# A new order for all five queues of a chunk-select attention with a gated MLP

## The chip, the cores and the metric

The kernel runs on one core of one Trainium2 chip. The metric is the device time in microseconds (us) of one execution.

## The reference

Four batches of 768 positions and 512 features. First an attention of 8 heads of 64, then an MLP block on its output:

```python
k_min, k_max = k_chunks.min(3), k_chunks.max(3)          # 24 chunks of 32 keys
ub = sum(maximum(q * k_min, q * k_max))                  # upper bound of q.k in a chunk
top_chunks = argsort(where(causal, ub, -1e9))[..., -6:]  # 6 chunks for each query
attn = softmax(where(sel & causal, q @ k.T / 8, -1e9)) @ v
x = attn with its heads side by side                     # (4, 768, 512)
u, v = split(gelu(x @ w_in))                             # 512 and 512
v_s = w_sg @ (layernorm(v) * g_ln) + b_sg                # over the 768 positions
out = x + (u * v_s) @ w_out                              # float32
```

## The kernel before

The program is written out by hand as 1267 operations. `_build` makes them in the order in which they are thought, each with its engine, a tag and what it reads and writes; `TABLE` then gives, for each of the five queues (PE, ACT, DVE, POOL, SP), the list of operation numbers in the order in which that engine runs them, the PSUM bank of each of PE's output tiles (`slots`), and the engine of those operations that can run on more than one (`engine`). `place` takes the lists as they are, `link` works out which waits on semaphores the order needs, and `emit` writes each queue. An engine runs its queue strictly in order: an instruction that waits holds up all that stand behind it on that engine.

The work goes by 16 pairs of heads (four pairs to a batch) and, behind each fourth pair, by batch. The tags that this text uses:

- Loads on SP's queue: `kn`, `qn`, `vn` (a pair's keys, queries, values, three buffers each). A buffer comes free when its last reader is done: that of `vn_11` with `vcast_8`.
- `kmm`, `kred` (L596, L613, DVE): minimum and maximum of each chunk of 32 keys; `wsub` (L601, DVE) makes the difference that the bounds product uses. `ktr`, `qtr` (PE) and `kev`, `qev` (ACT or DVE, L375 and L378): keys and queries turned and copied out of PSUM. `rel` (L375 on ACT, L377 on POOL and DVE): max(q, 0).
- `ub` (L696, PE): the upper bounds. `m8` (L713, L763), `dn` (L719, L768), `dt` (L723, L771), all DVE: the eight largest, the comparison of the bounds with the sixth, and the turning of its result; `qd` copies that result into the operand `QA` of the scores.
- `kcast`, `qcast`, `kcp`, `vcast`: casts to bf16 and copies, most of them on POOL (L378). `kT` (L623): the keys turned by a transposing transfer on SP's queue.
- `sc` (L812, PE) the scores, `exp` (L818, L873, ACT), `aff` (L823, POOL) the causal part of the mask on the diagonal blocks, `pv`, `pvd` (L896, L903, PE) the product with the values, `rcp` and `xs` (L911, L919) the division.
- `dt_x` (L927): the attention output turned by a transposing transfer on SP's queue, four for each of batches 1 and 2 and two for batch 3 (`dt_x_1_0` to `dt_x_1_3`).
- `hv`, `hu` (L950, L990, PE): the two halves of x @ w_in, with gelu on ACT (L954, L995). The layer norm of v is a chain on two engines: `bns`, `bna` (L959, L961, DVE) the statistics of six tiles, `var` (L963, DVE), `rstd` (L965, POOL, the power -0.5), `nmr` (L967, DVE), then six `vhat`, the normalised tiles, on ACT (L973) or DVE (L978).
- `pt` (L1007, PE): w_sg times `vhat`; each of its groups reads all six tiles. `vs`, `gt` (L1013, L1017, DVE): bias and gate. `ou` (L1030, PE), `os` (L1036, DVE), `st` (L1043, SP or ACT): w_out, the residual, the store.

A tag ends with the pair or batch and the part: `vhat_1_3` is tile 3 of batch 1, `qd_10_1` the second head of pair 10. The products of one batch are interleaved with the scores of the next batch's pairs, so all engines work on two or three pairs and a batch at once.

Of the kernel before, what the change touches and what calls it, by code (L numbers as in the profile page):

```python
# [258 lines left out]
def _build(nc, ctx, q, k, v, w_in, g_ln, w_sg, b_sg, w_out, out):  # L259
# [852 lines left out]
    for p in range(4, NP + 4):  # L1112
# [21 lines left out]

TABLE = {
# [15 lines left out]
    "act": (  # L1151
# [10 lines left out]
    "dve": (  # L1162
# [16 lines left out]
    "pool": (  # L1179
# [12 lines left out]
    "slots": (  # L1192
        "7314540635701767417545434327664501450123017623544450145016745767215354160145450101237305501452301450141"
        "3253136406153734136267206061520463145674567016732310123452345454774213567016723450104250167014523675763"
        "4121051765072355610147332155450467672345454554370167016723234216644167010123230123066767010167451752414"
        "3511004157267361266727074160101676723234301234523674575454523452367750012301014501435654023273353454272"
        "4540161502447"),
    "engine": (
# [10 lines left out]
}  # L1209


# [56 lines left out]
```

How the kernel before makes its waits and increments, by code:

```python
        def run(e, eng):  # L186
            for i in self.order[e]:
                o = ops[i]
                need = {}
                for d in o.waits:
                    p = ops[d]
                    s = dsem[p.dma] if p.dma is not None else sems[p.eng]
                    key = p.dma if p.dma is not None else p.eng
                    if key not in need or need[key][1] < p.count:
                        need[key] = (s, p.count)
                for s, c in need.values():
                    eng.wait_ge(s, c)
                ins = o.fn(eng)
                if o.dma is not None:
                    ins.then_inc(dsem[o.dma], 16)
                elif o.inc:
                    ins.then_inc(sems[e], 1)
            if e == "sp":
                for d, idxs in self.dma_sems.items():
                    if ops[idxs[-1]].tag[0] == "st":
                        eng.wait_ge(dsem[d], 16 * len(idxs))
```

## Time and profile before

| | us |
|---|---|
| median of 3 runs | 216.65 (216.13 to 218.79) |
| the profiled execution | 217.55 |
| its span, as the profile measures it | 215.4 |
| mean granted clock of TensorE | 0.992 of full speed |
| busy in that span: PE, DVE, ACT, POOL | 194.8, 185.5, 163.7, 132.8 |

The profile is that of one execution. Its rows give the start in the span and the duration in us; "xN" is the number of instructions that a row groups. A bracket at the end of a row holds the time for which the engine sat idle before it and, behind the arrow, the instruction that ended the wait. In a window's row the busy time of each engine stands ahead of its number of instructions; the granted clock is a share of full speed; a DMA share of 1 is all 16 DMA engines busy. SPq and ACTq are the queues that issue transfers; their rows last as long as the issue takes, not the transfer.

### The profile page before, as it was taken

To read this page: it belongs to the slowest core of one execution; us is meant where nothing else is said; L and a number is where in the kernel's file an instruction comes from. 1 tells how busy PE (TensorE), PEld (TensorE's weight loads), DVE (VectorE), ACT (ScalarE), POOL (GpSimd) and SP (SyncE) were. 2 spreads that over 40 slices of the span, in tenths; PEclk is the share of its full clock that TensorE was granted. 3 is DMA by queue.
4 is the path that set the end of the run, shared out by engine and by line. 5 is a ranking of instruction groups with operands and counts; after the bars stand their busy time and mean duration, and the time that the engine had idled before them with its cause. 6 is when DMAs were issued, how large, how long until landed. Compare 5 with 4: busy or idle time off the path is not lost.

```text
span 215.4 us, 6383 instructions
## 1 busy us (share of the span) xinstructions
PE 194.8 (90%) x2549; PEld 126.0 (58%) x2564; DVE 185.5 (86%) x531; ACT 163.7 (76%) x247; POOL 132.8 (62%) x168
## 2 busy tenths in 40 slices
PE   7778897899999999997959989998995999999993
PEld 2445676745766577763535757873572677655652
DVE  3899999798999999969889999987779664888994
ACT  3559998799999999977795889979685698765010
POOL 5447699798799999994596795987059016002000
PEclk9999999999999999999999999999999799999999
DMA  7999999999998999999895838698500213103117
GB/s 147 218 221 252 213 214 336 227 270 257 198 235 189 229 203 215 200 171 195 177 219 117 190 76 203 130 173 203 104 3 2 53 35 88 49 0 127 70 49 243
DMA packets 96801, 35.02 MB, mean 163 GB/s; under 512 B 91514, under 2 KB 92292, under 8 KB 96772
## 3 DMA queue, kind: packets, MB, share of 16 engines
q1 hardware_dynamic: 95908, 33.70, 73.5%
q10 hardware_dynamic: 864, 0.92, 1.3%
q8 instruction: 20, 0.33, 0.7%
q14 instruction: 9, 0.07, 0.1%
HBM read 24.38 MB, written 6.29 MB: 142 GB/s over the span
## 4 chain that ended last, share of the span: by engine, by line
PE 44%; DVE 35%; ACT 11%; issue 3%; DMA 3%; POOL 2%; SPq 0%; DVEq 0%
PE PS L1007 8%; PE PS L950 8%; PE PS L812 7%; PE PS L1030 7%; DVE PS L1013 3%; DVE vhat L978 3%; PE PS L896 3%; DVE Bn L613 3%; DVE uT L1017 3%; PE PS L990 3%; DVE XS L919 3%; ACT vgb L954 2%; ACT E L873 2%; PE PS L696 2%; DVE KA L378 2%
## 5 line engine op out<-in xcount | busy, mean ns | idle before, releaser
L818 ACT ACTIVATE E<-PS 128x1024 bf16<-128x1024 f32 (+1 forms) x72 | 62.3, 924 | 9.2 <-PE PS L812 8.5
L1007 PE MATMUL PS<-wsgT,vhat 128*128 128x384 bf16 x192 | 35.9, 334 | 5.1 <-DVE vhat L978 4.7
L812 PE MATMUL PS<-QA,KA 128*128 128x128 bf16 (+2 forms) x336 | 36.1, 247 | 0.4 <-DVE rden L911 0.3
L812 PEld LDWEIGHTS PS<-QA,KA 128*128 128x128 bf16 x336 | 23.9, 98 | 10.9 <-ACT E L818 1.8
L823 POOL TENSOR_SCALAR_AFFINE_SELECT E<-E 128x768 bf16<-128x768 bf16 x24 | 20.4, 864 | 13.5 <-ACT E L818 12.8
L1007 PEld LDWEIGHTS PS<-wsgT,vhat 128*128 128x128 bf16 x192 | 18.3, 100 | 17.3 <-issue 6.2
L378 POOL CAST QA<-qT 64x768 bf16<-64x768 f32 (+1 forms) x27 | 22.2, 826 | 7.1 <-DVE qT L378 3.8
L995 ACT ACTIVATE uT<-PS 128x384 bf16<-128x384 f32 x32 | 15.1, 505 | 12.8 <-PE PS L990 12.7
L990 PE MATMUL PS<-xT,winb 128*128 128x384 bf16 x128 | 23.1, 326 | 0.0
L950 PE MATMUL PS<-winb,xT 128*128 128x512 bf16 x92 | 20.8, 379 | 2.4 <-issue 0.9
L873 ACT ACTIVATE E<-PS 128x1024 bf16<-128x1024 f32 (+1 forms) x24 | 20.5, 926 | 2.6 <-PE PS L858 2.4
L1030 PE MATMUL PS<-woutb,uT 128*128 128x512 bf16 (+1 forms) x98 | 21.8, 353 | 0.6 <-issue 0.2
L1013 DVE SCALAR_TENSOR_TENSOR PS<-PS,bgT,bsgbc 128x384 f32<-128x384 f32 x32 | 19.2, 614 | 2.3 <-PE PS L1007 2.3
L965 POOL TENSOR_TENSOR rstd<-rstd,neghalf 128x6 f32<-128x6 f32 x4 | 5.4, 1348 | 24.8 <-DVE rstd L963 24.8
L896 PE MATMUL PS<-vx,E 128*128 128x65 bf16 x480 | 19.3, 194 | 0.4 <-issue 0.4
L959 DVE BATCH_NORM_STATS2 stats<-vgb 128x6 f32<-128x512 f32 x24 | 16.0, 683 | 3.9 <-ACT vgb L954 3.8
L613 DVE TRANSPOSE_TENSOR_REDUCE Bn<-kn 128x24 f32<-128x768 f32 x20 | 18.9, 957 | 0.0
L1036 DVE TENSOR_TENSOR osb<-PS,XS 128x512 f32<-128x512 f32 x21 | 14.2, 681 | 4.9 <-PE PS L1030 3.2
L896 PEld LDWEIGHTS PS<-vx,E 128*128 128x128 bf16 x480 | 16.9, 98 | 2.0 <-issue 0.8
L1017 DVE TENSOR_TENSOR uT<-PS,uT 128x384 bf16<-128x384 f32 x32 | 17.4, 550 | 0.6 <-ACT uT L995 0.2
L990 PEld LDWEIGHTS PS<-xT,winb 128*128 128x128 bf16 x128 | 12.1, 98 | 8.6 <-ACT vgb L954 0.2
L919 DVE TENSOR_TENSOR XS<-PS,rden 128x384 bf16<-128x384 f32 x30 | 16.3, 550 | 0.5
(121 smaller groups left out, 388.3 us busy)
## 6 DMA issues: line engine op xcount, KB each, us to landing
qn<-in_q_dram SPq DMA_DIRECT2D x32, 192.0 KB, 5.2
vn<-in_v_dram SPq DMA_DIRECT2D x16, 384.0 KB, 5.3
out_dram<-osb SPq DMA_DIRECT2D x20, 256.0 KB, 2.6
kn<-in_k_dram SPq DMA_DIRECT2D x10, 384.0 KB, 5.9
kn<-in_k_dram SPq DMA_DIRECT2D x12, 192.0 KB, 4.5
uT<-in_moe_w_sg_dram SPq DMA_DIRECT2D x4, 384.0 KB, 5.9
vgb<-in_moe_w_in_dram SPq DMA_DIRECT2D x3, 512.0 KB, 7.7
vhat<-in_moe_w_sg_dram SPq DMA_DIRECT2D x2, 384.0 KB, 3.8
```

Of the source, the lines that this page charges most:

```text
L378: return e.tensor_copy(dst(), src())
L613: P.op("dve", lambda d, m=m, op=op: d.tensor_reduce(Bn[u][:, x, m, :], kn[s][:].rearrange("p i t d -> p (i t d)").rearrange("p (c x) -> p ...
L812: r = e.matmul(both(ts)[:, o:o + n], KA[w][i][:, 128 * kb:128 * kb + 128], QA[w][i][:, q0:q0 + n], start=True, stop=True)
L818: P.op("act", lambda e, ts=ts, c0=c0, c1=c1, i=i: e.activation(E[es][:, i, c0:c1], both(ts)[:, 0:c1 - c0], ACTF.Exp, scale=SCALE), act(c1 ...
L873: P.op("act", lambda e, ts=ts, c0=c0, c1=c1, n=n: e.activation(E[es][:, :, c0:c1], both(ts).rearrange("p (i x) -> p i x", i=2)[:, :, 0:n], ...
L896: r = e.matmul(t.ap()[:, 65 * qb:65 * qb + 65], E[es][:, i, a:a + 128], vx[w][:, kb, i, :], start=first, stop=False, skip_group_check=True)
L950: r = e.matmul(t.ap()[:, 0:F], xT[s][:, dk, 128 * qt:128 * qt + 128], winb[:, dk, F:DFF], start=(dk == 0), stop=(dk == NDK - 1))
L990: r = e.matmul(t.ap()[:, 0:TG], winb[:, dk, 128 * fb:128 * fb + 128], xT[s][:, dk, TG * tg:TG * tg + TG], start=(dk == 0), stop=(dk == NDK ...
L1007: r = e.matmul(t.ap()[:, 0:TG], vhat[s][:, sb, 128 * fb:128 * fb + 128], wsgT[:, sb, TG * tg:TG * tg + TG], start=(sb == 0), stop=(sb == N ...
L1013: P.op("dve", lambda d, t=t, fb=fb, tg=tg: d.scalar_tensor_tensor(t.ap()[:, 0:TG], t.ap()[:, 0:TG], bgT[:, NT + fb:NT + fb + 1], bsgbc[:, ...
L1017: P.op("dve", lambda d, t=t, fb=fb, tg=tg: d.tensor_tensor(gT[s][:, fb, TG * tg:TG * tg + TG], t.ap()[:, 0:TG], uT[s][:, fb, TG * tg:TG * ...
L1030: r = e.matmul(t.ap()[:, 0:c1 - c0], gT[s][:, fb, 128 * qt:128 * qt + 128], woutb[:, fb, c0:c1], start=(fb == 0), stop=(fb == NF - 1))
```

## The change

Only `TABLE` changes. The operations themselves are the same 1267, with the same operands and tiles. The lists of all five queues stand in a new order, PSUM banks are given anew to the tiles, and the engine of 74 operations changes: 18 from POOL to ACT, 15 from ACT to DVE, 14 from ACT to POOL, 14 from DVE to ACT, 6 from DVE to POOL, 4 from POOL to DVE, and three stores of the last batch from ACT's queue to SP's. The queues hold 338, 235, 403, 164 and 127 operations before (PE, ACT, DVE, POOL, SP), 338, 235, 402, 162 and 130 after. At the same place in their queue stand 85 of PE's, 24 of ACT's, 53 of DVE's, 16 of POOL's, 23 of SP's; the others move by 1, 3, 2, 3 and 2 places in the median and by at most 15, 17, 50, 31 and 20.

The lists are rows of numbers; the lines of DVE and POOL around the layer norms of batches 1 and 2 (735 is `var_1`, 736 `rstd_1`, 737 `nmr_1`, 738 to 743 `vhat_1_0` to `vhat_1_5`, 1007 `rstd_2`):

```diff
-        "593 595 510 688 699 698 700 687 695 713 717 714 718 721 696 725 722 726 729 733 730 734 735 697 737 743 742 "
-        "740 741 701 686 761 702 762 782 767 783 788 768 764 765 705 789 791 792 770 875 822 823 826 771 692 690 693 "
...
+        "510 685 688 699 698 695 700 717 829 713 714 721 718 725 722 726 729 696 733 730 734 735 697 701 737 741 740 "
+        "742 739 686 702 782 783 687 761 788 767 762 764 789 768 765 791 792 875 770 822 771 823 692 677 690 693 876 "
...
-        "418 657 353 635 539 396 619 626 664 578 606 681 584 607 540 824 674 637 643 579 736 644 815 547 683 870 638 "
-        "704 833 832 863 682 586 645 684 808 703 913 853 827 872 906 677 846 948 922 865 871 834 893 866 957 941 964 "
-        "930 965 894 1086 1109 873 1007 1079 977 978 931 980 932 1102 966 960 1125 1149 1156 1132 967 1192 "),
...
+        "545 353 396 626 619 664 657 608 606 578 683 674 643 607 584 637 824 540 547 638 863 644 736 704 684 605 703 "
...
+        "929 965 1086 1079 1109 924 925 873 980 966 977 1007 1125 1102 1132 979 1156 1149 967 1192 "),
```

The same with tags, for the places that the prediction comes to ("..." for what lies between):

```
DVE, pairs 0, 1    before  ... utr_0_0 m8_0_0 init_13 dn_0 wsub_1_1 wsub_1_0 dt_0 ...
                   after   ... wsub_1_0 utr_0_0 wsub_1_1 m8_0_0 dn_0 qev_2_0 dt_0 ...
rel_0, rel_1       before  on ACT        after  on POOL
first loads of SP  the same 34 in both orders, qn_0 issued 2nd and 4th, before 4th and 5th
SP, batch 1        before  dt_x_1_0 st_0_1 dt_x_1_1 dt_x_1_2 dt_x_1_3 kT_10 vn_8
                   after   kT_10 kn_13 qn_12_1 dt_x_1_0 dt_x_1_1 dt_x_1_2 dt_x_1_3 vn_8
                           (st_0_1 earlier)
SP, vn_11          before  vn_8 qn_13_0 qn_13_1 qn_14_0 kn_14 qn_14_1 vn_10 st_0_5 vn_9 kn_15 kT_11 vn_11
                   after   vn_8 qn_13_0 kT_11 qn_15_0 qn_14_1 qn_13_1 kn_14 qn_14_0 vn_11
POOL, batch 1      before  kcast_12 kcast_11 kcp_10_1 qcast_10_0 kcp_9_0 rstd_1 qcast_10_1 aff_8_1 vcast_8
                           qcast_11_1 rel_13 kcp_10_0 qd_10_1 ... vcast_11
                   after   kcast_12 kcp_8_0 vcast_8 kcp_10_0 kcast_13 qcast_10_1 rstd_1 qd_10_1 vcast_11 qd_8_0
DVE, batch 1       before  var_1 m8_10_0 nmr_1 vhat_1_5 vhat_1_4 vhat_1_2 vhat_1_3 dn_10 kred_12_1 ... dt_10
                   after   var_1 m8_10_0 dn_10 nmr_1 vhat_1_3 vhat_1_2 vhat_1_4 vhat_1_1 kred_12_1 ... dt_10
PE, batch 1        before  pt_1_0_0 pt_1_1_0 pt_1_0_2 sc_9_1_1 sc_8_0_1 pt_1_1_2 pt_1_0_1 sc_8_0_2
                   after   sc_9_1_1 pt_1_1_0 pt_1_0_0 pt_1_1_2 pt_1_0_2 sc_8_0_2
SP, batch 2        before  dt_x_2_2 dt_x_2_3
                   after   dt_x_2_2 kT_15 st_1_1 kT_14 dt_x_2_3
POOL, batch 2      before  rstd_2 aff_12_0 qd_14_0 qd_14_1 qcast_14_1 qd_15_1 vcast_14 aff_13_0 qcast_15_1
                   after   vcast_13 qd_15_1 qcast_15_1 qd_14_0 rstd_2 aff_14_0 aff_13_0 aff_14_1
DVE, batch 2       before  bna_2_4 bna_2_5 var_2 dt_14 nmr_2 and four vhat_2 (3, 1, 5, 4)
                   after   dt_14 ... bna_2_5 bna_2_4 var_2 nmr_2 and four vhat_2 (0, 5, 3, 2)
PE, batch 2        after   all six hv_2 ahead of the first hu_2
```

## Rows read from the trace of the kernel before

**Rows 1.** The page's first part: busy us (share of the span) and instructions of each engine.

```profile
PE 194.8 (90%) x2549; PEld 126.0 (58%) x2564; DVE 185.5 (86%) x531; ACT 163.7 (76%) x247; POOL 132.8 (62%) x168
```

**Rows 2.** Windows: stretch, length, engines' busy us (count), granted clock, DMA share, GB/s.

```profile
0.00:44.00 44.00, 36.55 (x678) 24.06 (x681) 37.59 (x125) 32.49 (x45) 30.74 (x50) 1.00 1.09 226
62.50:99.00 36.50, 34.78 (x607) 24.05 (x608) 34.43 (x108) 33.29 (x46) 32.98 (x40) 1.00 1.10 201
99.00:112.60 13.60, 10.95 (x67) 5.77 (x68) 11.94 (x41) 11.28 (x22) 9.20 (x11) 1.00 0.97 207
162.00:164.00 2.00, 0.00 (x0) 0.00 (x0) 2.00 (x3) 1.97 (x4) 1.83 (x3) 1.00 0.00 0
165.95:169.36 3.41, 3.41 (x18) 1.95 (x17) 2.29 (x6) 1.01 (x6) 1.43 (x2) 0.50 0.00 0
```

**Rows 3.** Chain of waits, around both gaps of the middle: start, us, engine, work.

```profile
96.29 2.83 DMA xT<-XS
...
108.70 3.87 DVE vhat L978 x4
...
160.51 3.52 DVE vhat L978 x4
```

**Rows 4.** Timeline of PE; in brackets the idle time before and who ended it.

```profile
13.83 0.69 PE L696 MATMUL PS<-qT,Wall 64*32 64x288 f32 x8 [1.26 <-DVE Wall L601]
...
99.39 1.46 PE L950 MATMUL PS<-winb,xT 128*128 128x512 bf16 x6 [0.89 <-DMA xT<-XS]
...
112.71 3.08 PE L1007 MATMUL PS<-wsgT,vhat 128*128 128x384 bf16 x18 [2.37 <-DVE vhat L978]
...
164.17 1.14 PE L1007 MATMUL PS<-wsgT,vhat 128*128 128x384 bf16 x6 [2.32 <-DVE vhat L978]
...
165.78 1.98 PE L1007 MATMUL PS<-wsgT,vhat 128*128 128x384 bf16 x6 [0.29 <-DVE XS L919]
```

**Rows 5.** Groups by line and shape: busy us, mean ns | idle time before.

```profile
L377 POOL TENSOR_SCALAR rT<-qT 128x576 f32<-128x576 f32 x8 | 13.9, 1735 | 0.9 <-DVE Wall L649 0.4 <-POOL QA L378 0.3
...
L375 ACT ACTIVATE rT<-qT 128x576 f32<-128x576 f32 x7 | 4.8, 713 | 0.8 <-DVE qT L378 0.7
```

**Rows 6.** Timeline of SP's queue, batch 1: start, us to issue, line, transfer.

```profile
93.22 4.35 SPq L927 DMA_TRANSPOSE xT<-XS  x3
97.61 1.29 SPq L623 DMA_TRANSPOSE KA<-kbx  x1
...
116.87 0.57 SPq L539 DMA_DIRECT2D vn<-in_v_dram  x1
```

**Rows 7.** Timeline of DVE around the three normalisations and one compare.

```profile
56.05 0.72 DVE L768 TENSOR_TENSOR Dn<-U,m 128x576 bf16<-128x576 f32 x1
...
159.66 0.81 DVE L967 SCALAR_TENSOR_TENSOR nmr<-mv,rstd 128x6 f32<-128x6 f32 x1 [0.79 <-POOL rstd L965]
160.51 3.52 DVE L978 TENSOR_SCALAR vhat<-vgb,mv,rstd 128x512 bf16<-128x512 f32 x4
...
195.50 1.92 DVE L978 TENSOR_SCALAR vhat<-vgb,mv,rstd 128x512 bf16<-128x512 f32 x4
```

**Rows 8.** Timeline of POOL around rstd of batches 0, 1 and 2.

```profile
55.34 1.35 POOL L965 TENSOR_TENSOR rstd<-rstd,neghalf 128x6 f32<-128x6 f32 x1 [1.84 <-DVE rstd L963]
...
107.10 1.36 POOL L965 TENSOR_TENSOR rstd<-rstd,neghalf 128x6 f32<-128x6 f32 x1 [2.28 <-DVE rstd L963]
108.52 0.83 POOL L378 CAST QA<-qT 64x768 bf16<-64x768 f32 x1
...
111.38 0.90 POOL L378 CAST QA<-qT 64x768 bf16<-64x768 f32 x1
...
158.28 1.35 POOL L965 TENSOR_TENSOR rstd<-rstd,neghalf 128x6 f32<-128x6 f32 x1 [8.63 <-DVE rstd L963]
...
160.52 1.46 POOL L378 COPY QA<-Dt 32x576 bf16<-32x576 bf16 x2
```

**Rows 9.** The page's DMA issues, loads of v: count, KB each, us to landing.

```profile
vn<-in_v_dram SPq DMA_DIRECT2D x16, 384.0 KB, 5.3
```

More of the change, by code:

```diff
@@ L1136 @@
     "pe": (
[14 rows of a table removed]
-    "act": (
[9 rows of a table removed]
[14 rows of a table added]
+    "act": (
[9 rows of a table added]
         "1266 1251 "),
     "dve": (
[16 rows of a table removed]
-    "pool": (
[12 rows of a table removed]
-    "slots": (
[L1193 to L1197, printed above, removed]
-    "engine": (
[10 rows of a table removed]
[16 rows of a table added]
+    "pool": (
[12 rows of a table added]
+    "slots": (
+        "7254656104434567504750772235464501012301677623016016701016745325470430630145450101017052723452367450110"
+        "0632431631273611473015324140741676101452367016757500123236701455667542367010123450107236701452345456213"
+        "0167411761064565137546367356757401230101014567322323012301454227105445010123230123546767670167453253544"
+        "0732021663474654776725266760101456723675701014501014563010123234545723014523234501504140357004712753102"
+        "4132546056116"),
+    "engine": (
[10 rows of a table added]
 }
```

111 rows, old and new, of the table TABLE are left out of this document.

## The prediction

> **What bounds the kernel now.** I read the busy shares first [rows 1]: TensorE (PE) is busy for 194.8 of 215.4 us, so a new order of the same work can only win back what PE loses in some 20 us of gaps, or keep the other engines from being the ones that make them. The profiled execution took 217.55 us: 215.4 us of span and 2.15 us around it. The sum below is made against 217.55; the median of the three runs, 216.65, lies 0.90 below it, and I carry that 0.90 over at the end.
>
> The stretches come next [rows 2]. Here the reader is to see that the gaps have places. In the first 44 us PE is busy for 36.55, at a DMA share of 1.09, so this stretch is fed by transfers that are already back to back. From 62.5 to 99 us PE, DVE, ACT and POOL are all busy for over 32.9 of 36.5 us: here every order meets a full engine. The rest comes down to two places in the middle: 99 to 112.6, where PE misses 2.65 us, and 162 to 164, where PE does nothing at all while DVE (2.00), ACT (1.97) and POOL (1.83) are all full. Behind the second gap stands a stretch of 3.41 us in which PE works without a pause at a granted clock of 0.50.
>
> The chain of waits [rows 3] says who holds the end at these places: a transposing transfer (xT) of batch 1, and twice the four DVE instructions `vhat` (the normalisation of v, line 978), 3.87 and 3.52 us. PE's own timeline [rows 4] prices the waits: 1.26 us at 13.83 for `Wall`, 0.89 at 99.39 for xT, 2.37 at 112.71 and 2.32 at 164.17 for `vhat`, and 0.29 at 165.78.
>
> **The change, part by part.** Instructions and bytes are the same but for 74 that run on another engine; by their groups' mean durations that is +0.8 us for ACT, -0.3 for DVE and -3.2 for POOL, against the busy times of [rows 1] nothing that bounds. So each term is a wait that appears or goes. The last digit of a name is the part of it (`vhat_1_3`: batch 1, tile 3; `kT_10`: head pair 10).
>
> 1. *Head.* The wait of 1.26 us [rows 4] is for `wsub_1`, which stands on DVE behind a top-8, a mask operation and a compare of pair 0; the new order puts it ahead of them: at best -1.25. Against it, `rel_0` and `rel_1` go from ACT to POOL, 1735 ns instead of 713 [rows 5], so the bounds product that needs them is ready up to 1.0 later (+1.0). The first 34 loads are the same set in both orders and the DMA share is full, so the end of the stretch can't come much earlier whatever PE does. I take half of the gain, **-0.6, between -1.25 and +1.0**.
>
> 2. *xT of batch 1.* hv of batch 1 waits for the last of four `dt_x_1` on SP's queue, which issues them from 93.22 with no gap [rows 6]; `kT_10`, 1.29 us, stood behind them and now stands ahead of all four. hv is late by that unless SP finds a gap before: **+1.0, between 0 and +1.29**.
>
> 3. *`vhat` of batch 1.* Four of them took 3.87 us from 108.70 and 3.52 from 160.51 [rows 3], but 1.92 from 195.50 [rows 7]. What differs is POOL [rows 8]: four casts and selects lie beside the first (108.52, the last at 111.38), two copies and more beside the second (160.52), nothing beside the third. In the new order the instruction behind `rstd_1` on POOL is `qd_10_1`. It needs `dt_10`, which stands on DVE behind the four `vhat`; so POOL must stand idle while they run. They end 3.87 - 1.92 = 1.95 earlier, and PE's first product that reads them has a score group (`sc_9_1_1`, moved ahead) to fill what is left of the 2.37: **-2.0, between -2.4 (the whole wait and no more) and 0**. Where the cover goes: the casts that stood beside `vhat` now stand ahead of `rstd_1`, which is term 4.
>  The compare `dn_10` also moves, from behind the `vhat` to between `m8_10_0` and `nmr_1`, so it runs beside `rstd_1`. Cost 0: `dn` of an earlier pair ran at 56.05 beside `rstd_0` (55.34 to 56.69) in 0.72 us, with `rstd_0` no longer than the others (1.35; 1.36 at 107.10) [rows 7, 8]. The Trainium skill, "SBUF — State Buffer", section "Who interferes with whom", says that a DVE instruction with two inputs in SBUF and a GpSimd instruction that reads SBUF lock each other out for a whole instruction; by that rule `dn_10` and `rstd_1` would run one after the other, and the sum would be -4.4. These two rows overlap by 0.64 us, so by them the trace doesn't agree for this pair, though by term 3's rows it does for `vhat`.
>
> 4. *`rstd_1` on POOL* now has four casts and copies ahead of it that stood behind or elsewhere (`vcast_8`, `kcp_10_0`, `kcast_13`, `qcast_10_1`), 0.83 us each by the row at 108.52, 3.3 in all. POOL sat idle for 2.28 us ahead of `rstd_1` [rows 8], which leaves 1.0; some of the four can run earlier still: **+0.4, between 0 and +0.9**.
>
> 5. *hv of batch 2.* On SP `kT_15` and `kT_14` (1.29 each by the one at 97.61 [rows 6]) now lie ahead of the last `dt_x_2`. The first can hide in a queue that is slack there; the two can't both: **+0.4, between 0 and +1.3**.
>
> 6. *`vhat` of batch 2.* Behind `rstd_2` POOL now has three causal selects that wait for exponentials, which ACT can give only after the gelus of this batch and a change of its table; the two selects, two copies and two casts that stood there go ahead of `rstd_2`, into 8.63 us in which POOL waited [rows 8], or behind. So POOL is idle beside these four as well: 3.52 - 1.92 = 1.6, and `nmr_2`, 0.81 for six numbers in a row [rows 7], lay beside a select and falls by some 0.6. `dt_14` leaves the place ahead of `nmr_2`, and all hv now come before all hu, so the statistics end earlier. Together that exceeds the wait of 2.32 and the one of 0.29 at 165.78 [rows 4], so both go whole: **-2.6, between -2.6 and 0**.
>
> 7. *Clock.* The 3.41 us at 0.50 [rows 2] come right behind the 2 us in which PE did nothing. Without the gap they would take half: **-1.7, between -1.7 and 0**.
>
> 8. *Elsewhere.* Between the named places the instructions move by one to three places in the median, in stretches that are full: 0. The most to win in 62.5 to 99 is DVE's 2.07 us of idle time [rows 2]; the most to lose at one new wait is what the largest old one in such a stretch costs, 1.26 [rows 4]. The tail is 0: three stores go from ACT's queue to SP's, the last chain (product, add, store) is the same.
>
> Sum: -0.6 + 1.0 - 2.0 + 0.4 + 0.4 - 2.6 - 1.7 = **-5.1**, so 217.55 - 5.1 = 212.45 for an execution like the profiled one, and **211.5** for the median.
>
> **The rivals.**
>
> *POOL in order, waiting for a load.* `vcast_11` now stands ahead of `qd_8_0`, which the score group `sc_8_0_2` needs and PE reaches near 115.6 (110.7 for the first product of batch 1, then five groups at some 1 us, as the 18 matmuls from 112.71 are three in 3.08 [rows 4]). The load of vn_11 was issued at 116.87 [rows 6] and such loads land 5.3 us later [rows 9]: 122.2, and with the cast (0.83) and the copy (half of the 1.46 at 160.52) 123.8: PE stands for 8.2 us. 211.5 + 8.2 = 219.7, and if the clock falls to 0.50 behind such a gap as it did at 165.95, 1.7 more: **219.7 to 221.4**, slower than before. For it: POOL is in order, and vn_11 sits in a buffer that is free only after `vcast_8`, which is itself late on POOL. Against it: on SP the load stands ahead of a store and three loads that preceded it before. It decides if vn_11 lands after about 114.
>
> *The transfers take it back.* Terms 1, 2, 4 and 5 all at their upper ends: +1.0, +1.29, +0.9, +1.3 in place of -0.6, +1.0, +0.4, +0.4, which is +3.3: **214.8**. For it: SP issues without a gap before 99.4, and the loads run at a share over 1 up to then [rows 2]. Against it: four upper ends at once.
>
> *The gaps are refilled.* What PE wins at 112 and 164 it waits for at the next product, since DVE was busy for 11.94 of 13.60 us ahead of the first and full in the second [rows 2], and its work is the same: **216.6**, no change. Against it: DVE's own time falls here, as the `vhat` get shorter by 3.5 us.
>
> *`dn_10` and `rstd_1` one after the other.* If they shut each other out as `vhat` and the casts seem to, `nmr_1` is late by the 0.72 us of a compare, and so are the `vhat`: **212.2**. For it: the `vhat` rows; against it: the overlap of 0.64 us at 56.05. The page's rule of term 3 is this case.
>
> **How the numbers follow.** A median more than 2% off, which is about what a measurement of this kernel can tell from no change, is below 212.3 or above 221.0. The forecast has 0.47 and a range of its own from 208.0 to 213.5: the low end is terms 1, 3, 6 and 7 at their lower and 2, 4 and 5 at zero, -7.95, so 208.7, and 0.7 for the spread of the runs (the fastest of the three lies 0.52 below the median). Of the 0.47, 0.43 lies below 212.3. The compare beside `rstd_1` has 0.11, half of it (0.06) below 212.3; the transfers have 0.19, the refilled gaps 0.11, the load behind POOL 0.12, half of it above 221.0. Faster 0.43 + 0.06 = 0.49; same 0.04 + 0.05 + 0.19 + 0.11 + 0.06 = 0.45; slower 0.06. The range leaves out the slow rival (0.12) and little else: 208.0 to 216.8.
>
> **What would show it.** Terms 3 and 6: the four `vhat` rows near 1.9 us with no POOL row beside them, and PE's waits for `vhat` under 0.5. Term 7: no stretch of 0.50 near 166. Term 1: no wait for `Wall` near 13.8. Terms 2 and 5: a wait of PE for xT at the first hv of batches 1 and 2, longer than 0.89 in batch 1. Term 4: `rstd_1` starting more than 0.2 us after its variance. The slow rival: a wait of several us near 115 for a POOL copy to QA. It would be wrong if the `vhat` stay long with POOL idle, or if the time won at 112 is lost again before 149.

## The result and the profile after

The changed kernel took **209.28 us** (median of 4 runs, 207.63 to 211.59) beside 216.43 for the kernel before: a ratio of 0.9621, interval 0.9521 to 0.9722. The forecast was 211.5 in a range of 208.0 to 216.8. Two more sets of four runs of the same kernel gave 210.48 (0.9764, 0.9723 to 0.9804) and 210.92 (0.9745, 0.9686 to 0.9804), so all twelve have a median of 210.5: about 6 us under before, where the sum was 5.1. The ratios are those of the fast runs alone and so not the quotients of the medians, and the profile of a_cover1, told below, is of a slow run (219.30 us against that kernel's median of 214.70), so only its waits are read. The profiled execution below is the fastest of the twelve, 207.63 us with a span of 205.6; where it flatters the change, the later profiles say so.

Page of the changed kernel, first part, as [rows 1]:

```profile
PE 191.6 (93%) x2564; PEld 124.8 (61%) x2564; DVE 177.7 (86%) x530; ACT 163.3 (79%) x245; POOL 129.2 (63%) x166
```

Windows, columns as [rows 2]; the first two lie where rows 2 have a gap of PE, the third covers the head:

```profile
99.00:112.60 13.60, 13.52 (x88) 7.43 (x86) 12.03 (x35) 11.94 (x22) 6.29 (x8) 1.00 1.10 226
149.30:166.00 16.70, 16.70 (x174) 11.44 (x173) 13.87 (x34) 14.70 (x23) 5.43 (x8) 1.00 0.01 2
0.00:44.00 44.00, 36.31 (x684) 24.53 (x685) 36.32 (x125) 35.24 (x50) 33.69 (x52) 1.00 1.08 229
```

PE misses 0.08 us in the stretch where it missed 2.65, and nothing from 149.3 to 166, at full clock: both gaps of the middle are gone, and so is the stretch at 0.50 (1.2 of TensorE's 2.4 GHz). The wait for xT, which lay in part inside the first window, now lies ahead of it (below). The head is as it was (36.31 against 36.55 us busy).

Chain of waits, as [rows 3]:

```profile
95.10 2.82 DMA xT<-XS
98.01 3.63 PE PS L950 x16
105.72 1.36 POOL rstd L965
```

The `vhat` have left the chain's long pieces; the transfer of xT is still there.

Timeline of PE, as [rows 4]:

```profile
13.91 0.69 PE L696 MATMUL PS<-qT,Wall 64*32 64x288 f32 x8 [0.18 <-POOL rT L377]
...
98.01 1.24 PE L950 MATMUL PS<-winb,xT 128*128 128x512 bf16 x5 [2.28 <-DMA xT<-XS]
...
109.59 4.06 PE L1007 MATMUL PS<-wsgT,vhat 128*128 128x384 bf16 x24
...
156.70 3.57 PE L1007 MATMUL PS<-wsgT,vhat 128*128 128x384 bf16 x21
```

The first products of batches 1 and 2 (109.59, 156.70) wait for nothing. The wait of 1.26 us for `Wall` is now one of 0.18 for POOL's `rel_1`, at the same time of day (13.91 against 13.83). The wait for xT has grown from 0.89 to 2.28.

Timelines of DVE and POOL, as [rows 7, 8]:

```profile
106.31 0.76 DVE L768 TENSOR_TENSOR Dn<-U,m 128x576 bf16<-128x576 f32 x1
107.11 0.17 DVE L967 SCALAR_TENSOR_TENSOR nmr<-mv,rstd 128x6 f32<-128x6 f32 x1
107.32 1.92 DVE L978 TENSOR_SCALAR vhat<-vgb,mv,rstd 128x512 bf16<-128x512 f32 x4
...
154.63 1.92 DVE L978 TENSOR_SCALAR vhat<-vgb,mv,rstd 128x512 bf16<-128x512 f32 x4
...
185.89 1.92 DVE L978 TENSOR_SCALAR vhat<-vgb,mv,rstd 128x512 bf16<-128x512 f32 x4
```

```profile
105.72 1.36 POOL L965 TENSOR_TENSOR rstd<-rstd,neghalf 128x6 f32<-128x6 f32 x1 [1.74 <-DVE rstd L963]
110.84 0.65 POOL L378 COPY QA<-Dt 32x576 bf16<-32x576 bf16 x1 [3.76 <-DVE Dt L771]
111.56 0.82 POOL L378 CAST vx<-vn 128x768 bf16<-128x768 f32 x1
...
153.05 1.35 POOL L965 TENSOR_TENSOR rstd<-rstd,neghalf 128x6 f32<-128x6 f32 x1 [2.89 <-DVE rstd L963]
```

All three sets of four `vhat` take 1.92 us. POOL is idle beside the first two: 3.76 us ahead of `qd_10_1` (110.84), nothing behind `rstd_2` at 153.05 until 162. `dn_10` (106.31) ran inside `rstd_1` (105.72 to 107.08) in 0.76 us, and `nmr_1` followed 0.03 us behind `rstd_1`.

SP's queue, as [rows 6]: `kT_10`, then, behind a load of keys and one of queries (`kn_13`, `qn_12_1`), the four `dt_x_1`.

```profile
85.70 1.22 SPq L623 DMA_TRANSPOSE KA<-kbx  x1
...
90.05 6.34 SPq L927 DMA_TRANSPOSE xT<-XS  x4
```

To see which stages moved, I count along PE's queue, which has 338 operations in either order: the table gives the time between the ends of its operations 159, 174, 189, 204, 264 and 279, from the traces of the kernel before, of three executions of the changed one and of three experiments told below (b_head differs from before by two moves on DVE). At each of these places the two orders have run the same operations but for at most one. The stages are the head, batch 0 and the attention of batch 1; hv of batch 1; its hu and its first products; its next products among scores; up to the end of hu of batch 2; the first products of batch 2; the rest.

| | to 159 | 174 | 189 | 204 | 264 | 279 | 338 |
|---|---|---|---|---|---|---|---|
| before | 93.3 | 12.3 | 13.5 | 8.7 | 33.3 | 13.5 | 37.6 |
| b_head | 96.6 | 11.1 | 13.5 | 8.7 | 33.2 | 11.9 | 37.6 |
| changed | 91.5 | 13.0 | 10.6 | 7.6 | 33.3 | 9.0 | 37.5 |
| a_again | 94.9 | 12.8 | 10.7 | 7.6 | 33.5 | 9.0 | 37.5 |
| a_again2 | 94.8 | 12.8 | 10.6 | 7.6 | 33.5 | 8.9 | 37.5 |
| b_pool2 | 93.9 | 11.1 | 14.9 | 8.6 | 33.5 | 9.3 | 37.6 |
| b_three | 93.8 | 11.0 | 11.2 | 8.6 | 33.8 | 9.3 | 37.6 |

From the third column on, executions of one kernel agree within 0.2 us, but for stretches at half the clock (before at 279; b_pool2 at 189). The changed order wins 2.8 at 189, 1.1 at 204, and 3.0 at 279 (against 11.9; the 13.5 holds the stretch at 0.50 as well). It loses 0.5 to 2.0 at 174, behind xT. The first column varies by 3 us between executions of one kernel (91.5 to 94.9), more than the orders differ.

### The profile page after: what moved, and what is told of

Same layout as the page of the kernel before. It is cut to its first block, busy times and chain, and to the rows that moved or that the text cites. A ratio compares the mean times of both kernels' runs of the same rounds, so it can differ in the third digit from the quotient of the medians.

```text
span 205.6 us, 6389 instructions
## 1 busy us (share of the span) xinstructions
PE 191.6 (93%) x2564; PEld 124.8 (61%) x2564; DVE 177.7 (86%) x530; ACT 163.3 (79%) x245; POOL 129.2 (63%) x166
## 4 chain that ended last, share of the span: by engine, by line
PE 56%; POOL 14%; DVE 13%; ACT 7%; issue 4%; DMA 3%; SPq 1%; POOLq 0%; DVEq 0%
PE PS L950 10%; PE PS L1007 9%; PE PS L812 8%; PE PS L990 7%; PE PS L1030 5%; POOL QA L378 5%; PE PS L896 5%; ACT E L873 4%; POOL E L823 3%; PE PS L743 2%; PE PS L567 2%; DMA qn<-in_q_dram 2%; DVE uT L1017 2%; PE PS L903 2%; DVE PS L1013 2%
## 5 line engine op out<-in xcount | busy, mean ns | idle before, releaser
L1007 PE MATMUL PS<-wsgT,vhat 128*128 128x384 bf16 x192 | 34.2, 326 | 0.0
L950 PE MATMUL PS<-winb,xT 128*128 128x512 bf16 x96 | 21.7, 379 | 3.0 <-DMA xT<-XS 2.3
L1030 PE MATMUL PS<-woutb,uT 128*128 128x512 bf16 (+1 forms) x108 | 24.0, 355 | 0.0
L995 ACT ACTIVATE uT<-PS 128x384 bf16<-128x384 f32 x32 | 14.0, 489 | 10.4 <-PE PS L990 10.3
L378 POOL CAST QA<-qT 64x768 bf16<-64x768 f32 (+1 forms) x24 | 20.2, 842 | 3.0 <-DVE qT L378 1.2
L378 POOL COPY QA<-Dt 32x576 bf16<-32x576 bf16 x23 | 15.2, 662 | 8.1 <-DVE Dt L771 6.3
L954 ACT ACTIVATE vgb<-PS 128x512 f32<-128x512 f32 x24 | 13.8, 594 | 6.5 <-PE PS L950 6.3
L950 PEld LDWEIGHTS PS<-winb,xT 128*128 128x128 bf16 x96 | 9.0, 98 | 14.2 <-issue 2.9
L919 DVE TENSOR_TENSOR XS<-PS,rden 128x384 bf16<-128x384 f32 x31 | 16.8, 546 | 0.5
```

Of the source, the lines that this page charges most:

```text
L378: return e.tensor_copy(dst(), src())
L950: r = e.matmul(t.ap()[:, 0:F], xT[s][:, dk, 128 * qt:128 * qt + 128], winb[:, dk, F:DFF], start=(dk == 0), stop=(dk == NDK - 1))
L1007: r = e.matmul(t.ap()[:, 0:TG], vhat[s][:, sb, 128 * fb:128 * fb + 128], wsgT[:, sb, TG * tg:TG * tg + TG], start=(sb == 0), stop=(sb == N ...
L1030: r = e.matmul(t.ap()[:, 0:c1 - c0], gT[s][:, fb, 128 * qt:128 * qt + 128], woutb[:, fb, c0:c1], start=(fb == 0), stop=(fb == NF - 1))
```

## Experiments

Numbers in the diffs are operations, as in the change. Labels with a_ start from the changed kernel, with b_ from the kernel before.

**1. The changed kernel again** (a_again, a_again2; no edit).

> The changed kernel once more, unchanged, beside the other runs. The profiled execution of it took 207.63 us at a granted clock of 0.999, two others 209.18 and 209.38 at 0.992. Theory: the 1.6 us between them is one stretch of some 3.4 us at half the clock, which comes in some executions and not in others; so a run here lies near 207.6 or near 209.3, and a profile at 0.992 shows one stretch at 0.50 behind a wait of PE. Rival: the runs at 209.3 wait for transfers somewhere, and their lower clock is spread over the span: then no single stretch at 0.50.

> The changed kernel unchanged, as the measure for the other three runs beside it. Expected 209 to 211 us, 2.3 to 3.5 per cent under the kernel before, and in the profile PE's wait for xT at the first hv of batch 1 between 1.5 and 2.8 us.

Measured: 210.48 and 210.92. Both profiles have a clock of 0.991 or 0.992. Windows of the first (columns as before), and its PE timeline:

```profile
8.00:10.00 2.00, 0.65 (x13) 0.48 (x12) 1.32 (x6) 0.84 (x2) 1.91 (x1) 1.00 1.35 218
...
12.00:14.00 2.00, 2.00 (x16) 0.55 (x8) 0.55 (x3) 1.54 (x3) 1.65 (x1) 0.50 1.35 218
```

```profile
101.21 5.12 PE L950 MATMUL PS<-winb,xT 128*128 128x512 bf16 x23 [2.08 <-DMA xT<-XS]
```

One stretch at 0.50, as the theory had it, but in the head, behind 8 to 10 us in which PE was busy for 0.65 of 2.00 us. The theory's price failed: all eight runs lie between 210.00 and 211.48, and two of them (210.26 and 210.00) had a clock of 1.0, so the clock alone does not part 207.63 from the others. Against the fastest execution a_again's PE is 1.0 us late at its 17th operation, behind that stretch, and 3.4 at its 159th; what made the other 2.4, at full clock, is open. And the wait for xT stands at 101.21, 3.2 us later than in the fastest execution, since PE came to it that much later.

**2. POOL's work put back beside `vhat` of batch 2** (a_cover2).

```diff
 pool
-924 925 873 980 966 977 1007 1125
+924 873 1007 925 980 966 977 1125
```

> The changed kernel with four of POOL's copies and casts (kcp_14_0, qd_15_1, qcast_15_1, qd_14_0, some 3 us) moved from ahead of rstd_2 to behind it, so that they lie beside the four vhat of batch 2 again; nothing else. My theory (a vhat on DVE and a cast or copy on POOL shut each other out): the four vhat go from 1.92 us to between 3.2 and 3.8, PE waits 1.3 to 1.9 us ahead of the first product of batch 2, the time is up by that, and by 1.7 more if the clock falls behind the wait. Rival (the gain of batch 2 came from the statistics, which end earlier because all hv stand ahead of hu): vhat stay under 2.3 or PE does not wait, and the time is up by less than 0.5 us.

Measured: 212.48, 2.0 above the a_again measured beside it. DVE, POOL and PE:

```profile
158.48 0.17 DVE L967 SCALAR_TENSOR_TENSOR nmr<-mv,rstd 128x6 f32<-128x6 f32 x1 [1.47 <-POOL rstd L965]
158.69 3.51 DVE L978 TENSOR_SCALAR vhat<-vgb,mv,rstd 128x512 bf16<-128x512 f32 x4
```

```profile
158.51 0.83 POOL L378 COPY KA<-INDF 64x768 bf16<-64x768 bf16 x1
...
161.17 0.74 POOL L378 COPY QA<-Dt 32x576 bf16<-32x576 bf16 x1
```

```profile
162.34 3.90 PE L1007 MATMUL PS<-wsgT,vhat 128*128 128x384 bf16 x23 [1.47 <-DVE vhat L978]
```

Four copies and casts on POOL, and the same `vhat` take 3.51 us; PE waits 1.47, both inside the theory's numbers. The time, up by 2.0, is 0.1 above the theory's 1.9, and the stage of the table's column 279 took 10.5 us against 9.0. So the earlier statistics alone don't carry the gain.

**3. The same for batch 1** (a_cover1, then a_cover1b).

```diff
 pool, a_cover1
-547 638 863 644 736 704
+547 736 638 863 644 704
 pool, a_cover1b
-824 540 547 638 863 644 736 704
+824 547 644 736 540 638 863 704
```

> The changed kernel with three of POOL's copies and casts (kcp_10_0, kcast_13, qcast_10_1, 2.5 us) moved from ahead of rstd_1 to behind it, beside the four vhat of batch 1; nothing else. My theory: the four vhat 3.0 to 3.6 us instead of 1.92, PE's first product of batch 1 waits for them some 1.0 to 1.5 us, time up by 1.0 to 1.5. Rival (the gain of batch 1 came from the score group that now stands ahead of the products, or from hv): vhat may get longer, but the time stays within 0.5 us.

Measured: 214.70, 4.2 above a_again, three times what I expected; the profile names the rest. ACT, then PE:

```profile
116.76 0.49 ACT L375 ACTIVATE qT<-PS 128x384 f32<-128x384 f32 x1 [3.79 <-POOL QA L378]
```

```profile
117.69 2.49 PE L990 MATMUL PS<-xT,winb 128*128 128x384 bf16 x8 [3.05 <-ACT uT L995]
```

The moved `qcast_10_1` frees the tile that ACT's next copy (`qev_13`) writes. ACT stood 3.79 us for it with the gelus behind, and PE 3.05 us for those. That the kernel's other runs have the same waits is inferred, from the next run, which has neither these waits nor a loss of that size. There I took this cast out:

> As a_cover1, but kcp_8_0 in place of qcast_10_1 goes behind rstd_1 (with kcp_10_0 and kcast_13), so that nothing moved frees a buffer that ACT or PE wait for. Theory (a_cover1 lost 1.0 to 1.5 us to the longer vhat and the rest to ACT, which waited 3.79 us for qcast_10_1): vhat of batch 1 about 3.3 us, PE waits 1 to 1.5 us, and the time is up by 1.0 to 1.6 against a_again's 210.48, not by 4.

Measured: 210.23 (209.11 to 211.75), no loss seen against 210.48 (another set of runs of before, 216.41 beside 216.32). DVE and PE:

```profile
107.70 3.32 DVE L978 TENSOR_SCALAR vhat<-vgb,mv,rstd 128x512 bf16<-128x512 f32 x4
```

```profile
111.17 4.06 PE L1007 MATMUL PS<-wsgT,vhat 128*128 128x384 bf16 x24 [0.88 <-DVE vhat L978]
```

The lock-out is there (3.32 us), the wait is 0.88 rather than 1.0 to 1.5, and a median of four runs that spread over 2.6 us can't show it. In the profile the stage of column 189 took 11.7 us against 10.6, so the loss is there, at the low end of the theory's 1.0 to 1.6. The `vhat` grew by 1.40 and the wait by 0.88; hu and a score group cover the difference.

**4. Casts added where there were none** (a_vhat3).

```diff
+    for n in range(4):
+        P.op("pool", lambda g: g.tensor_copy(kbx[0][:].rearrange("p i t -> p (i t)"), qT[0][:]), gps(S), ("junk", n),
+             reads=[("qT", 0, 0), ("qT", 0, 1)], writes=[("kbx", 0)])
 pool
-1192
+1192 1267 1268 1269 1270
```

> The changed kernel with four casts of 128x768 float32 to bf16 added on POOL right behind rstd_3, reading a tile that is done with and writing another, so that they lie beside the four vhat of batch 3, where POOL had nothing to do; their result is used by nothing. Theory: the four vhat go from 1.92 to 3.3 to 3.9 us, as those of batches 1 and 2 did beside other casts, and PE's first product of batch 3 is late by 1.4 to 1.9; nothing behind it can give that back: time up by that. Rival (the vhat of batches 1 and 2 were long for another reason, such as the transfers or the scores beside them): 1.92 to 2.3 us, time up by under 0.4.

Measured: 212.02, 1.5 above a_again. DVE, POOL, PE, and the window behind:

```profile
186.51 0.77 DVE L967 SCALAR_TENSOR_TENSOR nmr<-mv,rstd 128x6 f32<-128x6 f32 x1 [0.85 <-POOL rstd L965]
187.32 3.49 DVE L978 TENSOR_SCALAR vhat<-vgb,mv,rstd 128x512 bf16<-128x512 f32 x4
```

```profile
186.44 3.63 POOL L1133 CAST kbx<-qT 128x768 bf16<-128x768 f32 x4
```

```profile
190.95 8.66 PE L1007 MATMUL PS<-wsgT,vhat 128*128 128x384 bf16 x42 [2.07 <-DVE vhat L978]
```

```profile
190.00:195.00 5.00, 4.05 (x16) 2.03 (x17) 3.06 (x6) 0.00 (x0) 0.07 (x1) 0.70 0.01 3
```

From 1.92 to 3.49 us with nothing else changed. Even `nmr_3`, six numbers to a row, took 0.77 beside the first cast and takes 0.17 without. PE's wait of 2.07, where the changed kernel has none, is a little over the theory's 1.4 to 1.9, and was followed by a stretch at a lower clock, as in [rows 2].

**5. One part alone on the kernel before** (b_pool2).

```diff
 pool
-873 1007 1079 977 978 931 980 932 1102 966 960
+873 1079 977 978 931 980 966 932 1007 1102 960
 dve: 976 (dt_14) from ahead of 1008 to behind 975
```

> The kernel before with one part of the change alone: on POOL aff_12_0, qd_14_0, qd_14_1, qcast_14_1, qd_15_1, qcast_15_1 and vcast_14 moved ahead of rstd_2, and on DVE dt_14 moved to behind dn_14, since the copies read it. My theory: the four vhat of batch 2 fall from 3.52 to about 1.9 us, nmr_2 from 0.81 to 0.2, PE's wait of 2.32 us at the first product of batch 2 falls under 0.5, the stretch at half the clock goes: 2 to 4 us faster than before. Rival (the order of hv and hu is needed too): PE still waits over 1.5 us, and the time is within 1 us of before.

Measured: 213.39, ratio 0.9881 (0.9830 to 0.9931), 2.9 under before. DVE and PE:

```profile
160.54 0.17 DVE L967 SCALAR_TENSOR_TENSOR nmr<-mv,rstd 128x6 f32<-128x6 f32 x1 [1.47 <-POOL rstd L965]
160.75 1.92 DVE L978 TENSOR_SCALAR vhat<-vgb,mv,rstd 128x512 bf16<-128x512 f32 x4
```

```profile
112.09 4.24 PE L1007 MATMUL PS<-wsgT,vhat 128*128 128x384 bf16 x16 [2.37 <-DVE vhat L978]
...
162.81 1.14 PE L1007 MATMUL PS<-wsgT,vhat 128*128 128x384 bf16 x6
```

Eight operations moved, and batch 2's gain is there: 162.81 waits for nothing. The row at 112.09 is the untouched batch 1: same wait of 2.37, and this time the clock fell behind it (16 matmuls in 4.24 us; 18 took 3.08 in [rows 4]).

**6. Three parts together** (b_three).

```diff
 pool, besides b_pool2
-579 736 644 815 547 683 870 638 704 833
+579 644 547 736 704 815 683 870 638 833
 dve, besides b_pool2
-697 737 743 742 740 741 701 686 761 702 762
+697 701 737 743 742 740 741 686 702 761 762
-823 826 771 692 690 693 691 876
+823 692 690 693 691 826 771 876
```

> The kernel before with three local moves only: the one of b_pool2 for batch 2 (213.39 beside 216.32); the like for batch 1 (POOL: qcast_10_1 and vcast_8 ahead of rstd_1, qd_10_1 right behind it; DVE: dn_10 ahead of nmr_1, dt_10 behind kred_12_1); and on DVE the four small steps of the bounds of pair 12 (wcp_12, wsub_12) ahead of kcp_12_1 and gt_1_0_3, as PE waited 0.82 us for them at 126.61. Theory (the gain of the change is these three waits, and nothing comes from the rest): vhat of batch 1 1.92 us, PE's waits at 112.7 and 126.6 under 0.5 each, time 5 to 6 us below before, that is within 1 us of the changed kernel. Rival (a large part comes from the order everywhere else): at most 4 us below before.

Measured: 211.55, ratio 0.9795 (0.9703 to 0.9887): 4.9 under before, between the two theories' numbers and nearer to the first; some 1 us above the changed kernel. The interval, 2.4 to 6.4 us, holds both theories; the table decides, with 2.3 won at 189 (13.5 to 11.2) and 2.6 at 279 (11.9 to 9.3). DVE and PE:

```profile
107.80 1.92 DVE L978 TENSOR_SCALAR vhat<-vgb,mv,rstd 128x512 bf16<-128x512 f32 x4
```

```profile
109.87 3.08 PE L1007 MATMUL PS<-wsgT,vhat 128*128 128x384 bf16 x18 [0.41 <-DVE vhat L978]
...
123.09 0.36 PE L903 MATMUL PS<-vx,E 128*128 128x65 bf16 x6 [0.67 <-POOL E L823]
...
126.79 0.61 PE L812 MATMUL PS<-QA,KA 128*128 128x384 bf16 x4 [0.80 <-DVE U L752]
```

The `vhat` of batch 1 take 1.92 us, and the wait for them fell to 0.41. The wait for the bounds of pair 12 went too, but 0.67 and 0.80 us of other waits (for a select on POOL, for DVE's transposes) took its place, so the table's column 204 stays at 8.6: that third move gained nothing.

**7. The head alone** (b_head).

```diff
 dve
-82 63 64 20 65 86 83 66
+82 83 63 86 64 20 65 66
```

> The kernel before with DVE's wsub_1_0 moved ahead of utr_0_0 and wsub_1_1 ahead of m8_0_0, as in the change; nothing else. Term 1 of the prediction gave this move 0.6 to 1.25 us. My reading of the dependences now: the bounds of pair 1 also need rel_1, which ends 13.56 where wsub_1 ends 13.78, so PE's wait of 1.26 us falls by 0.2 to 0.3 alone and the time stays within 0.5 of before. Rival (term 1): the wait falls under 0.3, the time by 0.6 or more.

Measured: 217.08, ratio 1.0019 (0.9984 to 1.0054). PE, the end of `wsub_1` on DVE, and `rel_1` on ACT:

```profile
13.71 0.69 PE L696 MATMUL PS<-qT,Wall 64*32 64x288 f32 x8 [1.12 <-DVE Dn L719]
```

```profile
11.86 0.13 DVE L601 TENSOR_TENSOR Wall<-PS,Wall 128x12 f32<-128x12 f32 x1
```

```profile
12.88 0.68 ACT L375 ACTIVATE rT<-qT 128x576 f32<-128x576 f32 x1
```

`wsub_1` ended at 11.99 instead of 13.78, and PE still waited 1.12 us. In the program this product waits on `wsub_1` and `rel_1` alone, and `rel_1` ended at 13.55 before and 13.56 here; the row names another DVE instruction that happened to end last before it.

**8. kT_10 behind the transposes, and two repairs** (a_kT10, a_best, a_warm).

```diff
 sp, a_kT10
-647 636 673 648 552 612 650 710 421
+647 673 648 552 612 650 710 636 421
 sp, a_best
-647 636 673 648 552 612 650 710 421 707 675 896 837 708 835
+647 673 648 552 612 650 710 707 708 636 421 675 896 837 835
 pe, a_best and a_warm
-4 80 89 62 5 117
+4 5 80 89 62 117
```

> The changed kernel with kT_10 on SP's queue moved back from ahead of the four dt_x_1 to behind them; nothing else. Theory (term 2: SP issues in order, so kT_10 makes xT late): dt_x_1_3 is issued some 1.2 us earlier, PE's wait at the first hv of batch 1 falls from 2.1 to 2.8 us to about 1.0 to 1.5, the time falls by 0.8 to 1.3 (more where the clock fell behind that wait). Rival (the last division, or ACT, holds xT back): the wait and the time stay within 0.4.

Measured: 210.13. PE:

```profile
98.75 2.53 PE L950 MATMUL PS<-winb,xT 128*128 128x512 bf16 x11 [1.08 <-DMA xT<-XS]
...
108.13 0.59 PE L567 MATMUL PS<-identF,qn 64*128 64x64 f32 x12 [1.43 <-DMA qn<-in_q_dram]
```

xT came 1.0 us sooner (1.08 in place of 2.1 to 2.3), and 1.43 us went at the next place, for a load of q that `kT_10` now held up. So the time stayed within the 0.4 us of the rival, though not for its reason.

> The changed kernel with the move of a_warm, and on SP qn_13_0, qn_13_1, kT_10 and vn_8 in this order behind the four dt_x_1, as a_kT10 turned its gain of 1.0 us at xT into a wait of 1.43 us for qn_13_1, which kT_10 and vn_8 had pushed back. Theory (the wait only moves on because these loads come late): PE waits 1.1 us or less for xT and under 0.4 for qn_13_1, time 0.7 to 1.5 below a_again2. Rival (the transfers are full up to 110 us, so that whatever goes first the last one is late): another wait takes its place, time within 0.5 of a_again2.

Measured: 211.71, 0.8 above a_again2. POOL, ACT and PE:

```profile
102.48 0.83 POOL L378 COPY KA<-KA 64x768 bf16<-64x768 bf16 x1 [3.59 <-DMA KA<-kbx]
...
105.80 0.83 POOL L378 CAST vx<-vn 128x768 bf16<-128x768 f32 x1 [0.72 <-DMA vn<-in_v_dram]
```

```profile
109.81 0.49 ACT L375 ACTIVATE qT<-PS 128x384 f32<-128x384 f32 x1 [2.31 <-POOL QA L378]
```

```profile
110.73 1.47 PE L990 MATMUL PS<-xT,winb 128*128 128x384 bf16 x8 [1.57 <-ACT uT L995]
```

PE waited 1.00 us for xT, and the load of q was in time; but POOL stood 3.59 us for `kT_10`, whose result `kcp_10_1` copies, and 0.72 more for `vn_8`. `qcast_10_1` behind them came late too, and ACT waited 2.31 us for that tile, as in a_cover1. Another wait took the place, as the rival said, though by a queue and not by full transfers.

> The changed kernel with one pair of PE's filler products (the fourth keep_warm, which works on nothing) moved from behind the bounds of pair 0 to directly behind the third; nothing else. In the changed kernel PE does nothing from 8.2 to 9.4 us and in three of the five profiles so far its clock fell to 0.50 from 11 to 14 us, in the kernel before and its variants (busy 1.79 to 2.00 of 2 us from 8 to 10) in none. Theory (the fall follows that gap): with 0.5 us of it filled the stretch at 0.50 comes less often or not at all, time down by up to 1. Rival (it needs more than that, or the fall has another cause): a stretch at 0.50 between 10 and 15 us is there as before, time the same within 0.5.

Measured: 210.04 beside 210.92, intervals 0.9655 to 0.9799 and 0.9686 to 0.9804: they overlap, nothing is shown. Its profile has no stretch at 0.50 in the head, that of a_best, with the same move, has one. The expectation's count was short: four of the seven profiles of the new order taken by then have that fall, between 10.8 and 15.2 us; with a_again2 it is five of eight without the move, and of the four of the old order none.

## Why the forecast was right, term by term

*Terms 3 and 6, `vhat`* (-2.0 and -2.6): right in mechanism, and they are the change. a_cover2, a_cover1b and a_vhat3 make the long `vhat` at will (3.51, 3.32, 3.49) by POOL's work alone. Batch 1 gave 2.8 at column 189, of which term 4 should have taken 0.4; batch 2 gave 3.0 without the clock. b_three, with both and little else, has 4.9 of the 6 us. The rule that term 3 quotes from the Trainium skill ("SBUF — State Buffer", section "Who interferes with whom") is for a DVE instruction with two inputs in SBUF. `vhat` reads one tile and two columns of scalars, so that casts and copies hold it up stands on these runs and not on that rule.

*Term 2, xT* (+1.0): right in mechanism, and too small by most profiles. PE's wait grew from 0.89 to 2.06 to 2.28 in the three profiles, and `kT_10` accounts for 1.0 of it (a_kT10). But in b_head, b_pool2 and b_three, which keep the old order there, PE doesn't wait for xT at all, and column 174 is 1.7 to 2.0 below the changed kernel's, past the term's upper end of 1.29. `kn_13` and `qn_12_1` stand ahead of the four `dt_x_1` as well; no run moved these back.

*Term 4* (+0.4) and *term 5* (+0.4): too high. `rstd_1` ran at 105.72, 0.1 us behind its variance (105.46, 0.17 long), since the four casts had gone before; the first hv of batch 2 waited 0.53 to 0.78 us in the three profiles, for ACT's exponentials and not for xT, against 0.92 before.

*Term 1, head* (-0.6): wrong in mechanism. b_head shows that the wait named for `Wall` was held by `rel_1` as well. The row names the last of several releases; I read it as the only one.

*Term 7, clock* (-1.7): failed as put. The stretch at 0.50 of [rows 2] did go from that place. But of 34 runs of before 13 had a clock of 1.0 (median 215.44) and 16 one of 0.992 (216.61), while of the changed kernel's 12 only 3 had 0.999 or more. The change moved the falls, to the head above all, and did not clearly make them fewer. A term for the clock belonged in the range.

*Term 8, elsewhere* (0): the 1.1 us at column 204 stood outside the sum. It is in all three profiles of the new order. b_three's third move didn't reproduce it; which move makes it is open.

By the table 2.8 + 1.1 + 3.0, less 0.5 to 2.0 at xT and with the head within its noise, is 4.9 to 6.4 for the 6 of the medians. The forecast came near because two misses (1 and 7, 2.3 us too much) stood against 1.1 of term 8, 0.8 of terms 4 and 5 and 1.2 of `vhat` that it lacked.

*The rivals.* The load behind POOL: SP issued vn_11 from 105.07, against 116.87 in [rows 6], and `vcast_11` ran at 111.56 right behind `qd_10_1`; its kind of wait, an in-order POOL that holds ACT, is what a_cover1 and a_best built. The gaps were not refilled: column 264 is 33.3 in both orders, and DVE is busy for 7.8 us less (177.7 against 185.5), over twice the 3.5 that the argument against this rival counted on. The transfers' four upper ends didn't come together: terms 4 and 5 cost next to nothing.

The compare: `dn_10` beside `rstd_1` cost nothing in the changed kernel's profiles, where `rstd_1` began first (0.76 us, as long as one with no POOL row beside it, the first row here, from before). In a_kT10 `dn_10` began first, by 0.16 us, and `rstd_1` took 1.81 us instead of 1.36, so there the rival's mechanism is seen, at 0.45 us and off PE's path:

```profile
150.64 0.76 DVE L768 TENSOR_TENSOR Dn<-U,m 128x576 bf16<-128x576 f32 x1
```

```profile
107.06 0.76 DVE L768 TENSOR_TENSOR Dn<-U,m 128x576 bf16<-128x576 f32 x1
```

```profile
107.22 1.81 POOL L965 TENSOR_TENSOR rstd<-rstd,neghalf 128x6 f32<-128x6 f32 x1 [0.15 <-POOL QA L378]
```

The page "SBUF — State Buffer" of the Trainium skill, section "Who interferes with whom", has a DVE instruction with two SBUF inputs contend with a GpSimd instruction that reads SBUF: with a cast beside it `nmr_3` agrees (0.77 against 0.17); with `rstd` as the neighbour `dn_10` agrees in a_kT10 (1.81 against 1.36) and not in the changed kernel.

## What to carry to other kernels

Where the same DVE instruction takes twice as long at one place as at another, look at what POOL does beside it, and move POOL's work out of the span that ends a chain: eight moved operations gave half of this gain. Before such a move, list which tiles the moved instructions free and who writes them next, for an in-order queue passes the delay on to engines that the edit doesn't name. And a wait's row names one releaser; check when the others ended before pricing it.

## What the runs showed of the hardware

Four `vhat` on DVE took 1.92 us in every profile in which no POOL row lay beside them, and 3.32 to 3.87 us beside three to five POOL rows, most of them casts and copies.

A fall of the granted clock to 0.50 follows waits of PE of 0.8 to 2.4 us in some executions and not in others: behind the same 2.37 us at batch 1 there was none in the profile of before and one in b_pool2. The runs of before at a mean clock of 0.992, which fits one such stretch (half of 3.41 in 215.4 us), took 1.2 us more than those at 1.0 (216.61 against 215.44), less than the 1.7 that half of its 3.41 us gives.
